# Attention and FFN on one core: three buffers for the keys' operand, its sums' rows loaded a head further ahead, the maxima's rounds one a step

## What is computed

```python
# attention, for each of 4 batches and 8 heads
cum = np.cumsum(np.maximum(s, 0.0), axis=-1)
bias = -(cum[:, :, :, None] - cum[:, :, None, :])
scores = np.where(causal, -1e9, q @ k.T / 8 + np.minimum(bias, 0.0))
attn = np.exp(scores - scores.max(-1)); attn /= attn.sum(-1) + 1e-9
x = attn @ v                                   # heads side by side: 576 x 512
# first block
h = np.maximum(x @ w_in, 0.0)                  # 1024 channels
conv = conv_w[0] * h[s-1] + conv_w[1] * h[s] + conv_w[2] * h[s+1]
x = (h * sigmoid(conv)) @ w_out
# second block
u = x + (x.T @ U @ V).T                        # over the positions, rank 32
out = u + np.maximum(u @ w_ch1, 0.0) @ w_ch2   # 2048 channels between
```

## Time and profile before

| | us |
|---|---|
| median of 3 runs | 980.86 (978.79 to 982.56) |
| the profiled execution | 979.89 |
| its span, first to last instruction | 978.1 |
| TensorE busy in the span | 907.4 |
| VectorE busy | 491.6 |
| ScalarE busy | 350.9 |
| mean granted TensorE clock | 0.969 of full speed |

### The profile page before, as it was taken

One profiled execution on the slowest core, in us unless ns is written; L12 is line 12 of the kernel. 1 busy time (PEld: TensorE's weight loads), 2 busy tenths in 40 slices (PEclk: granted clock), 3 DMA queues, 4 the chain that ended last, 5 costly groups with the idle time before them and its releaser, 6 DMA issues.

```text
span 978.1 us, 15722 instructions
## 1 busy us (share of the span) xinstructions
PE 907.4 (93%) x6312; PEld 847.6 (87%) x6312; DVE 491.6 (50%) x876; ACT 350.9 (36%) x665; POOL 39.5 (4%) x82
## 2 busy tenths in 40 slices
PE   4777898988999999999899999999899999999998
PEld 3565787976999988988899998989899999999998
DVE  5464687535455783455443586154522591342222
ACT  2554465444332552444222344243422251221111
POOL 2011000000000000000000000000000000000000
PEclk9888798998999999999999999999999999999999
DMA  6655345661475434643454434532444444444441
GB/s 161 145 143 135 115 124 170 190 199 48 147 237 179 162 118 172 216 157 106 152 168 138 153 122 155 173 137 87 141 154 148 144 155 155 173 168 173 173 171 50
DMA packets 63280, 147.05 MB, mean 150 GB/s; under 512 B 29420, under 2 KB 43756, under 8 KB 50920
## 3 DMA queue, kind: packets, MB, share of 16 engines
q1 hardware_dynamic: 60904, 142.40, 45.1%
q0 software_dynamic: 2304, 3.65, 1.5%
HBM read 115.88 MB, written 30.09 MB: 149 GB/s over the span
## 4 chain that ended last, share of the span: by engine, by line
PE 76%; DVE 14%; ACT 4%; issue 3%; DMA 2%; SPq 1%; DVEq 0%; ACTq 0%
PE psum L1106 20%; PE psum L1108 19%; PE psum L1107 19%; PE psum L1085 7%; PE psum L1029 3%; PE psum L1062 2%; PE psum L1064 2%; DVE qb L804 2%; DVE kb L802 1%; DVE neg_max L817 1%; DVE work L877 1%; DMA kc<-cum_scratch 1%; DVE work L880 1%; PE psum L1069 1%; DVE work L875 1%
## 5 line engine op out<-in xcount | busy, mean ns | idle before, releaser
L1106 PE MATMUL psum<-uu_hl,ring 128*128 128x288 f32 x512 | 157.0, 307 | 9.8 <-DVE uu_hl L915 6.5
L1106 PE MATMUL psum<-r_hl,ring 128*128 128x288 f32 x512 | 155.4, 303 | 4.7 <-DVE u_acc L932 4.7
L1108 PE MATMUL psum<-uu_hl,ring 128*128 128x288 f32 x512 | 152.3, 297 | 0.0
L1107 PE MATMUL psum<-uu_hl,ring 128*128 128x288 f32 x512 | 152.0, 297 | 0.0
L1108 PE MATMUL psum<-r_hl,ring 128*128 128x288 f32 x512 | 151.2, 295 | 0.0
L1107 PE MATMUL psum<-r_hl,ring 128*128 128x288 f32 x512 | 151.0, 295 | 0.0
L1085 PE MATMUL psum<-probs,va 128*128 128x320 f32 (+4 forms) x448 | 125.8, 395 | 4.3 <-ACT probs L638 4.3
L920 DVE SCALAR_TENSOR_TENSOR r_hl<-psum,r_hl 128x288 fp32r<-128x288 f32 x128 | 58.4, 457 | 136.4 <-ACT r_hl L721 136.4
L721 ACT ACTIVATE r_hl<-psum 128x288 fp32r<-128x288 f32 x128 | 52.4, 410 | 191.6 <-PE psum L1108 191.6
L638 ACT ACTIVATE probs<-psum 128x320 f32<-128x320 f32 (+2 forms) x128 | 62.9, 501 | 136.9 <-PE psum L1069 110.7
L1106 PEld LDWEIGHTS psum<-uu_hl,ring 128*128 128x128 f32 x512 | 97.3, 190 | 13.4 <-DVE uu_hl L915 8.3
(11 more groups left out here) (100 smaller groups left out, 1693.3 us busy)
## 6 DMA issues: line engine op xcount, KB each, us to landing
ring<-w_scratch SPq DMA_DIRECT2D x72, 1024.0 KB, 4.8
w_scratch<-ring SPq DMA_DIRECT2D x24, 1024.0 KB, 5.0
kq_raw<-in_kq_t SPq DMA_DIRECT2D x64, 288.0 KB, 5.3
stage<-in_w_ch SPq DMA_DIRECT2D x16, 512.0 KB, 5.7
out_t<-u_acc SPq DMA_DIRECT2D x16, 288.0 KB, 3.5
va<-in_v SPq DMA_DIRECT2D x32, 128.0 KB, 2.2
spread_out<-few_scratch POOLq DMA_DIRECT2D x24, 144.0 KB, 3.1
stage<-in_w_in SPq DMA_DIRECT2D x4, 512.0 KB, 7.2
```

The costliest lines, as they stand in the source:

```text
L1106: pe.matmul(o, hi, m_hi, start=start, stop=False)
L1107: pe.matmul(o, hi, m_lo, start=False, stop=False)
L1108: return pe.matmul(o, lo, m_hi, start=False, stop=stop)
```

## The change

- `kc` has three buffers instead of two (`KCS`), with semaphores of their own. The sums' rows of head h+3 are now loaded at step 2 of head h. GpSimd sets the third buffer's constant rows at the start, and SyncE copies the first rows of three heads.
- TensorE makes chunks 0 and 1 of the scores together, ahead of the rounds of the maxima (`MAXIMA`). In bodies the rounds stand at steps 0, 1 and 2, and turning them to a row moves from step 3 to step 4 (`TURN`).
- In bodies the keys are prepared at step 2, high copy, second operand and low part, and the queries at step 3, behind the normalisation. In batch 0 both stay at step 3.
- In batch 0 the high part of a weight block moves to step 1 and the low part to step 2. The store and the raw load move from behind (1, 4), (2, 4), (4, 4) to behind (2, 1), (3, 1), (5, 1).
- `load_small` is in three parts, behind step 4 of heads 0, 1 and 2. U and V are split behind (3, 4).
- In bodies x is split at (3, 4), (5, 4) and (7, 4) instead of (4, 0), (6, 0) and (7, 4).

```diff
-        kc = [sb(f"kc{i}", [KROWS, S], F32R) for i in range(2)]
+        KCS = 3
+        kc = [sb(f"kc{i}", [KROWS, S], F32R) for i in range(KCS)]
...
-        SMALL_AT = (0, 4)
-        UV_AT = (2, 4)
+        UV_AT = (3, 4)
+
+        MAXIMA = [{0: (0, 1), 1: (2,)}, {0: (0,), 1: (1,), 2: (2,)}]
+        TURN = [3, 4]
...
-        X_SPLIT = {(4, 0): 0, (6, 0): 1, (7, 4): 2}
+        X_SPLIT = [{(4, 0): 0, (6, 0): 1, (7, 4): 2}, {(3, 4): 0, (5, 4): 1, (7, 4): 2}]
...
-                    mm_s.wait(sp, n - 2)
+                    mm_s.wait(sp, n - KCS)
...
                     if g == 2:
-                        load_cum(a, h + 2)
+                        load_cum(a, h + KCS)
...
-                    if (h, g) == SMALL_AT:
-                        load_small()
-                    if g == 4 and h in WEIGHTS_HEADS[:-1]:
-                        store_block(WEIGHTS_HEADS.index(h))
-                        load_raw(WEIGHTS_HEADS.index(h) + 2)
+                    if g == 4 and h < 3:
+                        load_small(h)
+                    if g == 1 and h - 1 in WEIGHTS_HEADS[:-1]:
+                        store_block(WEIGHTS_HEADS.index(h - 1))
+                        load_raw(WEIGHTS_HEADS.index(h - 1) + 2)
...
                 def attention_step(a, h, g):
+                    if g == TURN[a > 0]:
+                        max_to_row(a, h + 1)
                     if g == 3:
-                        max_to_row(a, h + 1)
-                        prepare(a, h + 2)
+                        if a == 0:
+                            prepare_keys(a, h + 2)
+                        prepare_queries(a, h + 2)
...
+                    if g == 2 and a:
+                        prepare_keys(a, h + 2)
...
-                    if g == 3 and h in WEIGHTS_HEADS:
+                    if g == 1 and h in WEIGHTS_HEADS:
                         weights_high(WEIGHTS_HEADS.index(h))
...
-                    if g == 3:
-                        highs(a, h + 2)
-                        lows(a, h + 2)
+                    if g == 3 and not a:
+                        key_high(a, h + 2)
+                        query_high(a, h + 2)
+                        key_low(a, h + 2)
+                        query_low(a, h + 2)
...
+                    if g == 2 and a:
+                        key_high(a, h + 2)
+                        key_low(a, h + 2)
+                    if g == 3 and a:
+                        query_high(a, h + 2)
+                        query_low(a, h + 2)
...
-                    if g == 4 and h in WEIGHTS_HEADS:
+                    if g == 2 and h in WEIGHTS_HEADS:
                         weights_low(WEIGHTS_HEADS.index(h))
...
                         scores(a, h, 0)
-                        max_scores(a, h + 1, 0)
                         scores(a, h, 1)
-                        max_scores(a, h + 1, 1)
-                    if g == 3:
+                    if g == TURN[a > 0]:
                         max_transpose(a, h + 1)
...
-                    if g == 1:
-                        max_scores(a, h + 1, 2)
+                    for r in MAXIMA[a > 0].get(g, ()):
+                        max_scores(a, h + 1, r)
```

More of the change, by code:

```diff
@@ L156, in attention_and_ffn_program @@
         v_in = [Count(sem(f"v_in{i}"), 32) for i in range(2)]
-        first_cum = [sem(f"first_cum{i}") for i in range(2)]
-        cum_in = Count(sem("cum_in"), 16)
+        first_cum = [sem(f"first_cum{i}") for i in range(KCS)]
+        cum_in = [Count(sem(f"cum_in{i}"), 16) for i in range(KCS)]
         s_in, cw_in, uv_in, cum_out = (sem(n) for n in ("s_in", "cw_in", "uv_in", "cum_out"))
@@ L519, in _ @@
                 load_v(0, 0)
-                for h in range(2):
-                    sp.wait_ge(s_rows1 if h else s_rows, 3)
+                for h in range(KCS):
+                    sp.wait_ge(s_rows1 if h else s_rows, 3 + 2 * (h > 1))
                     for x, done in enumerate((s_cumh, s_cuml)):
@@ L545, in _ @@
                     ffn_step(item)
-                cum_in.wait(sp, B * H - 3)
+                for n in range(B * H - KCS, B * H):
+                    cum_in[n % KCS].wait(sp, n // KCS - 1)
                 for c in (*raw_in, *v_in):
@@ L752, in ffn_step @@
                             weights_high(q)
-                prepare(0, 0)
-                prepare(0, 1)
+                for h in range(2):
+                    prepare_keys(0, h)
+                    prepare_queries(0, h)
                 max_to_row(0, 0)
@@ L786, in _, with key_high @@
                    .then_inc(s_cuml, 1)
[L788 removed]
+                def key_high(a, h):
                     n, i = a * H + h, h % 2
@@ L803, in lows, with query_low @@
                        .then_inc(kl_done.sem, 1)
+                def query_low(a, h):
+                    n, i = a * H + h, h % 2
+                    if n >= B * H:
+                        return
+                    prep_hi.wait(dve, n)
                     dve.scalar_tensor_tensor(out=qb[i][D:2 * D, :], in0=kq_raw[D:2 * D, i, 1, :], scalar=SCALE,
@@ L968, in ffn_step @@
                             weights_low(q)
-                highs(0, 0)
-                highs(0, 1)
-                lows(0, 0)
+                for h in range(2):
+                    key_high(0, h)
+                    query_high(0, h)
+                key_low(0, 0)
+                query_low(0, 0)
                 for r in range(len(ROUNDS)):
                     maxima(0, 0, r)
-                lows(0, 1)
+                key_low(0, 1)
+                query_low(0, 1)
                 for h, g in ATT_STEPS:
@@ L1014, in max_scores @@
                     if r == 0:
-                        pe.wait_ge(first_cum[n], 32) if n < 2 else cum_in.wait(pe, n - 2)
+                        pe.wait_ge(first_cum[n], 32) if n < KCS else cum_in[n % KCS].wait(pe, n // KCS - 1)
                         pe.wait_ge(copied.sem, copied.value(n))
```

52 lines of the change are left out of this document (31 added, 21 removed).

## The result

| | before | after |
|---|---|---|
| median, measured together | 979.83 (976.98 to 982.56, 4 runs) | 951.61 (947.39 to 954.09, 4 runs) |
| ratio to before, 95% interval | | 0.9708, 0.9661 to 0.9755 |
| profiled span | 978.1 | 948.6 |
| TensorE busy | 907.4 | 897.4 |
| mean granted clock | 0.969 | 0.977 |

The change takes 28 us off. The forecast was 959.

The account below looks back on a forecast made before the run. TensorE was followed, with 53 us of waits, and in batch 0 a loop through three engines as the bound. 979.9 less 9.2 (batch 0) and 12.3 (bodies) is 958.4; plus 1.0 for the runs' median, 959; range 943 to 974.

Parts of the forecast that it names:

- Batch 0: Head 0 to head 7 takes 71.3 us against 80.5, a gain of 9.2, between 5 and 19.
- The loop: In batch 0, ScalarE, VectorE and TensorE form a loop setting an undisturbed period of 8.12 us between heads' last exponentials.
- The spread copies: In batch 0, normalisations at heads 3 and 5 wait for late-landing copies, 2.8 and 3.7 us.
- The clock: In batch 0, two intervals with a long wait each lose 1.8 us to the lower clock, 3.6 in all.
- Rival B: Spread copies land in time in batch 0, which gains 6.5 and 3.6 us more: 949; chance 0.14.
- First body: Gains from the second operand, the turns and the clock: 2.7, 1.5, 2.0 and 1.0 us.
- Second and third body: Gains of 3.5 (accumulation), 2.0 (uu_hl) and 1.6 us (clock), less 2.0 for new waits.
- the new waits at (3, 4) and (5, 4): VectorE waits for ScalarE's high part of x, 0.5 us at each of four places, 2.0 charged.
- rival D: Slower: VectorE's wait for x's high part blocks evictions at five places, costing 20 us: 992; chance 0.06.
- Rival C: Bodies give nothing, VectorE's backlog only moves and waits reappear under other names: 971; chance 0.21.
- Rival E: Sums' rows are still late in batch 0, so 5 us come back: 964; chance 0.05.
- Rival F: No change to be told, Rival C with half of rival D: about 981; chance 0.06.

Follow-up runs that it names:

- e3_stores: Changed kernel with the second and third store and raw load one head later, behind (4, 1) and (6, 1): 948.60 us.
- e1_rows: Kernel before with only the third kc buffer and the sums' rows loaded one head earlier: 970.39 us.
- e2_batch0: Changed kernel with the bodies' four edits undone (maxima rounds, row's turn, keys' step, x split): 969.19 us.
- e12_after: Changed kernel measured again without any edit, giving its second trace: 953.65 us.
- e8_uv: e3_stores with U and V split behind (5, 2) instead of (3, 4), and GpSimd's clearing of hid behind the second pair: 945.14 us.
- e9_turn_split: e8_uv with the row of maxima turned at step 3 in the second and third body, step 4 in the first only: 940.24 us.
- e10_norm: e8_uv with batch 0's multiplications for pairs 0 and 1 behind (4, 2) and (6, 2), and x split at (5, 0) and (7, 0): 941.45 us.
- e11_both: e8_uv with the edits of both e9_turn_split and e10_norm: 935.80 us.
- e4_xsplit: Changed kernel with x split in bodies at (4, 0) and (6, 0) again: 953.87 us.
- e7_keys: Changed kernel with keys and queries in bodies both prepared at step 3 again: 966.46 us.

## Why the prediction was right, and where it wasn't

**Batch 0, predicted 9.2, measured 8.9 and 9.6.** The loop held: undisturbed intervals of 8.11 to 8.19, head 0 to 7 in 71.4 where 71.3 was predicted (70.2 in the second trace), the waits 2.70 and 3.56 where 2.8 and 3.7 were (2.87 and 2.73 in the second trace). Three things differ from its working.
- *The spread copies.* I took the issues at 7.5 behind the last exponential and the landings at 8.0 and 8.8. They were issued later (at 48.5 for head 2's 40.40, 8.1 behind, and at 73.2 for 64.40, 8.8 behind) and landed sooner (6.6 and 6.8 at most). The traffic delays both hops of the round trip, the transfer into `few_scratch` too. That the two errors cancel in the sum is luck.
- *The clock.* Predicted 3.6 in two intervals. 15.82 less 8.12, 2.52, 0.76 and 2.70 leaves 1.7; 14.14 less 8.12, 0.76 and 3.56 leaves 1.7; the last interval (8.89, with the small inverse in it) has 0.7 more. 4.1 in all, as a remainder.
- *Rival B* (the copies land in time) fell by the two rows of VectorE above. The Trainium skill, "DMA: Bandwidth & Descriptors", section "Queues, rings and completion order", has each DMA engine take turns between its queues, packet by packet; that this leaves no wait, as B concluded, is refuted by 2.70 and 3.56 us. The landings of 6.2 with the store and the raw load beside them and 3.4 without say that SyncE's transfers do hold up GpSimd's small copies here, by 2.8 us, less than the 6.5 and 8.6 us that the store and the load took to land. B's price was too high: with the second pair's wait gone and 0.90 of the first's left, `e3_stores` gained 5.4 in waits, where B has 6.5, and 1.6 of the clock's part, where B has 3.6.

**First body, predicted 7.2, measured 10.0 and 4.6.** The three traces with the old bodies (before, `e1_rows`, `e2_batch0`) have 200.5, 196.0 and 198.4, and the seven with the new ones (after, `e12_after`, `e3_stores`, `e8_uv`, `e9_turn_split`, `e10_norm`, `e11_both`) 190.5 to 195.9; the means are 198.3 and 192.6, a gain of 5.7. The term was about right, and a single trace could not have shown it. Step by step: the wait for the copies is 1.8 (predicted under 2), the turn's waits fell by 2.5 (predicted 2.0).

**Second and third body, predicted 5.1, measured 10.6 in both traces** (7.2 + 3.4 and 5.7 + 5.0). This is the term that was mis-sized, by half, and it is most of what lies between the forecast and the medians. TensorE's waits in these bodies before:

```profile
PE psum L1106 <- DVE u_acc L932: 7.0, 7, 1.8
PE psum L1106 <- DVE uu_hl L915: 4.4, 2, 2.2
...
PE psum L1106 <- DVE x_hl L845: 1.4, 2, 0.7
```

They idled 15.7 us in all and idle 7.6 now, 8.1 less. By name (the rows of the changed kernel stand at `e4_xsplit`):
- the waits for the accumulation fell from 7.0 to 3.1, where I took 3.5 (one of the eight of the earlier trace rows, 1.0 us, is in the first body);
- those for `uu_hl`, 2.21 in each body, fell by 3.2 in all, where I took 2.0;
- those for `x_hl` at the start of a body fell by 0.8, where I had no term;
- the new waits at (3, 4) and (5, 4), for which I charged 2.0, are real, and `e4_xsplit` puts them at 3.1. But the keys' move shortens the waits at the same places: 1.1 at (3, 4) as before, and 1.0 for 0.4 at (6, 0), which is in the 3.1 above. Beside the falls above nothing is left to charge. That is the step that failed: I took the row of 2.21 as the price of the new place, though it held VectorE's backlog with the keys' part in it, which the same change removes. `e7_keys` shows the mechanism of rival D, 2.26 instead of 1.1 at (3, 4), with that part put back. D needed 3 us at each of five places;
- of two stretches of 3.4 us at the lower clock one is left, at most 1.7, where I took 1.6. Some 0.8 of the 10.6 has no name.

**Rival C** (the bodies give nothing) is refuted by `e2_batch0`. **Rival E** (rows still late): no wait for them in any trace. **Rival F** fell with C and D.

The argument on VectorE held in kind: its work did not change (492.6 us busy against 491.6), and moving 1.2 us of it a step earlier, with ScalarE's copy, is worth 13 to 15 us in the changed kernel, 5.2 of them waits in the second and third body and much of the rest the clock behind these waits. What I had not seen is that undoing this one edit costs nearly the whole gain of the bodies; I had spread it over four. What the edit gives by itself, with the other three undone, no run shows.

## What to carry to other kernels

A wait's place is the sum of what stands in the queue ahead of it, so price a move by all waits behind the moved piece, the short ones too, add the stretches at the lower clock that go with them, and don't take a wait that the same change shortens as the price of a new one. A loop through three engines is best read by the distance between the same instruction of successive heads: its shortest value is the period, and each excess over it has a name in VectorE's or ScalarE's rows; work placed in the engine's own wait inside that loop is free or nearly so, as the weights, the normalisations and U and V were here (the last at 0.9, through one slow copy). Where a stage is compared by one trace each, take a second trace of the same kernel before a difference of 3 to 5 us is explained.

## What the runs showed of the hardware

- The same program with the same waits ran a stretch at 1.2 GHz in one execution and at 2.4 in another (0.52 and 1.00 behind the turns), which moved the first body by 5.4 us; the spans differ by 4.8. Without long waits in batch 0 the granted clock there was 0.99.
- Two small copies on GpSimd's queue landed in 3.4 us with only loads of keys beside them, and in 6.2 with a store and a load of weights issued on SyncE's queue 3 us earlier as well; the small transfer that precedes them was late by 1.4.
- Each of the four waits of 1.96 to 2.26 us on TensorE in the later bodies of `e7_keys` had a stretch at 1.2 GHz behind it (granted clock 0.50 over 3.3 and 6.6 us in the third body); of the four waits of 1.03 to 1.06 us at the same places of the changed kernel one had, 3.4 us long.
- A copy on VectorE that takes 0.45 us took 1.40 in four traces, each time beside a 1.06 us clearing on GpSimd.
